# Weight pieces loaded over the place of their low halves, an attention head issued in pairs, late pieces spread out, and a branch moved ahead of the last stores

## The chip, the cores and the metric

One NeuronCore of a Trainium2 chip runs the whole program in one launch. The metric is the device time of one execution in microseconds (us), lower is better. The kernel before takes 930.59 us, the median of three runs (928.19 to 931.43).

## The reference

```python
# q, k, v, f_logit: [4 batches, 8 heads, 768 steps, 48]
f = 1.0 / (1.0 + np.exp(-f_logit))
for t in range(S):                       # gated linear attention
    state = f[:, :, t, :, None] * state + np.einsum('bhd,bhe->bhde', k[:, :, t], v[:, :, t])
    y[:, :, t] = np.einsum('bhd,bhde->bhe', q[:, :, t], state)
# x = y as 3072 tokens x 384
h = x @ w_in                             # first MLP, 384 -> 2048 -> 384
g = np.where(h >= 1, h, np.where(h <= -1, 0.0, (h + 1) ** 2 / 4.0))
x = g @ w_out
h = x @ w2_in                            # second MLP, same sizes
g = (a[0] + a[1]*h + a[2]*h**2 + a[3]*h**3) / (1.0 + abs(b[0])*abs(h) + abs(b[1])*h**2 + 1e-06)
out = g @ w2_out
```

## The kernel before, in words

All data are float32. A large product is made of three rounded ones: each operand is split into a high half (`_hi`, a rounding copy made by ScalarE, ACT) and a low half (`_lo`, the difference, made by VectorE, DVE, or GpSimd, POOL), and TensorE (PE) multiplies high by high, high by low and low by high. Nine matmuls of 128x512 make one tile of a hidden layer from the 384 inputs, and nine add one hidden tile to the three output sums.

**Attention** is cut in 24 items (6 chunks of 128 steps by 4 groups of head pairs). For item i: ACT makes the gate (`gate_steps`), DVE a running product (`scan`), ACT its logarithm and exponential as a first inverse (`invert`), DVE refines it (`newton`) and scales the queries (`scale_queries`), POOL scales the keys (`scale_keys`), PE makes the scores, DVE masks them (`mask`), PE makes the outputs, transposes the keys and makes the change of state (`scores`, `outputs`, `transposes`, `deltas`), ACT and DVE split the result into `x_hi` and `x_lo` (`round_y`, `rest_y`), and DVE adds to the state (`states`). Items 0 to 3, which complete the inputs of the first 512 tokens, run in a head that is written out by hand.

**The first MLP** follows in 96 steps n (6 blocks of 512 tokens by 16 hidden tiles). Step n issues `spline_first(n)` (nine matmuls into one of two banks), ACT's relu and square (`spline_in`), DVE's join (`spline_join`), ACT's high half (`spline_hi`), DVE's low half (`spline_lo`), and two steps later `spline_second(n)` (nine matmuls). Item 4 + n//4 of attention is spread over four steps (a window): `transposes(i)` and `scores(i)` stand behind `spline_first` of the first step, `outputs(i)` and `deltas(i)` behind that of the third. `transposes(i)` waits until DVE has added the state change of item i-1.

**Weights.** Each MLP's weights are 16 pieces of 384 KB. They stay in `w_hi` and `w_lo` for all blocks. A raw piece is loaded by a DMA that SyncE (SP) issues into one of two buffers `w_raw`, ACT rounds it into `w_hi` (`split_w1`, `split_w2`), and POOL subtracts into `w_lo` in three parts. A load waits until POOL has finished with its buffer. The second MLP's pieces go to the same `w_hi` and `w_lo`, each as soon as the first MLP has read the old piece for the last time, in its last block (n from LAST_BLOCK = 80): ten at the steps in `STEPS2`, and six late ones at the steps 0 to 5 of the second MLP.

**The second MLP** has 48 units (6 blocks by 8), each of two hidden tiles: unit n's step issues `rational_first(n)` (18 matmuls) and `rational_second(n-4)` (18); ACT, DVE and POOL work between them. At the steps 4, 5 and 6 of a block POOL also makes one third of the next block's `x_lo` (`split_x2`), and `rational_first` of the next block waits for all three.

Each engine runs its own program in order, and semaphores tie them together, so the order in which the code is written decides what stands behind a wait. At the end a flag tells whether the fast path was valid. PE, DVE, ACT and SP read it (`value_load`), and each jumps over a long general program (`general`) that does not run here.

Of the kernel before, what the change touches and what calls it, by code (L numbers as in the profile page):

```python
# [58 lines left out]
ORDER1 = [m + UNITS * out for m in range(UNITS) for out in range(2)]  # L59
# [9 lines left out]
X2_STEPS = [3, 4, 6]  # L69

# [37 lines left out]
def build(nc, qT, kT, fT, vT, fC, kC, qC, vC, w1, w2, a, b, outT):  # L108
# [3 lines left out]
    with ctx:  # L112
# [9 lines left out]
        w_lo = lay.tile("w_lo", PIECES * WPC, F32R)  # L122
        x_hi = lay.tile("x_hi", [P, KT, 2 * NB], F32R)
# [3 lines left out]
        w_raw = [lay.tile(f"w_raw{u}", WPC) for u in range(2)]  # L127
# [105 lines left out]
        w1_loaded = [sem(f"w1_loaded{r}") for r in range(2)]  # L233
        w1_hi_done = sem("w1_hi_done")
        w1_lo_done = sem("w1_lo_done")
        w2_loaded = [sem(f"w2_loaded{r}") for r in range(2)]
# [94 lines left out]
        def _(sp):  # L331
# [32 lines left out]
            def load_w1(k):  # L364
                if k >= 2:
                    sp.wait_ge(w1_lo_done, SPLITS * (k - 1))
                at = ORDER1[k] * WPC
                sp.dma_start(w_raw[k % 2][:, :], w1[:, at:at + WPC]).then_inc(w1_loaded[k % 2], 16)

            def load_w2(k):  # L370
                if k >= 2:
                    sp.wait_ge(w2_lo_done, SPLITS * (k - 1))
                else:
                    sp.wait_ge(w1_lo_done, SPLITS * PIECES)
                at = ORDER2[k] * WPC
                sp.dma_start(w_raw[k % 2][:, :], w2[:, at:at + WPC]).then_inc(w2_loaded[k % 2], 16)
# [54 lines left out]
            load_f(5)  # L431
            move_fourth(0)
# [4 lines left out]
            load_w1(2)  # L437
            load_q(5)
            load_w1(3)
            load_v(5)  # L440
            load_w1(4)
            sp.dma_start(a_bc[:, :], a.rearrange("(o a) -> o a", o=1).to_broadcast([P, 4])).then_inc(coef_loaded, 16)
            sp.dma_start(b_bc[:, :], b.rearrange("(o a) -> o a", o=1).to_broadcast([P, 2])).then_inc(coef_loaded, 16)
            for n in range(N1):
# [10 lines left out]
                if n + HEAD_PIECES + 2 < PIECES:  # L455
                    load_w1(n + HEAD_PIECES + 2)
                if n % TILES == LAG1 + 1 and n >= TILES:
                    store1(n // TILES - 1)
                t = n - (N1 - TILES)
# [7 lines left out]
            for k in range(len(STEPS2) + 2, PIECES):  # L467
                load_w2(k)
# [5 lines left out]
            store2(BLOCKS - 1)  # L474
            sp.wait_ge(flag_set, 1)
            flag = sp.value_load(okflag[0:1, 0:1], min_val=0, max_val=P)
            sp.wait_ge(stored2, 16 * KT * BLOCKS)
            with sp.If(flag < P):
                general.sync_program(sp, qT, kT, fT, vT, xT, x1T, w1, w2, outT)

        @block.gpsimd
        def _(pool):
# [26 lines left out]
            def split_w1(k):  # L509
                pool.wait_ge(w1_hi_done, k + 1)  # L510
                for part in range(SPLITS):
                    own = slice(part * WPC // SPLITS, (part + 1) * WPC // SPLITS)
                    at = slice(ORDER1[k] * WPC + own.start, ORDER1[k] * WPC + own.stop)
                    nc.gpsimd.tensor_tensor(w_lo[:, at], w_raw[k % 2][:, own], w_hi[:, at].bitcast(F32),
                                            ALU.subtract).then_inc(w1_lo_done, 1)

            def split_w2(k):
                m = ORDER2[k]
                pool.wait_ge(w2_hi_done, k + 1)
                if m < UNITS:  # L520
                    pool.wait_ge(h1_ready, N1 - TILES + UW * (m + 1))
                else:
                    pool.wait_ge(multiplied1, N1 - TILES + UW * (m - UNITS + 1))
                for part in range(SPLITS):
                    own = slice(part * WPC // SPLITS, (part + 1) * WPC // SPLITS)
                    at = slice(m * WPC + own.start, m * WPC + own.stop)
                    nc.gpsimd.tensor_tensor(w_lo[:, at], w_raw[k % 2][:, own], w_hi[:, at].bitcast(F32),  # L527
# [37 lines left out]
            split_w1(1)  # L565
            scale_keys(4)
            split_w1(2)
# [449 lines left out]
        def _(pe):  # L1017
# [179 lines left out]
            for n in range(N1):  # L1197
                i, stage = window_of(n)
                spline_first(n)
                if n == 0:  # L1200
                    deltas(3)
# [298 lines left out]
```

## Time and profile before

| | us |
|---|---|
| median of 3 runs | 930.59 |
| the profiled execution, its whole time | 931.32 |
| its span in the profile | 929.6 |
| PE busy | 894.3 (96%) |
| DVE busy | 666.1 (72%) |
| ACT busy | 632.3 (68%) |
| POOL busy | 277.8 (30%) |
| ACT's last operation begins | 922.78 |

The span is the time from the first instruction to the last in one profiled execution, and 1.7 us lie around it. A busy PE is not PE at its peak: matmuls overlap in the profile, so the distance from one start to the next says more than the busy time.

### The profile page before, as it was taken

The numbers are of one execution on the slowest core, as the hardware profiler recorded it, in microseconds if no ns is written. First come the engines' busy times: TensorE is split into PE (matmuls) and PEld (weight loads), VectorE is DVE, ScalarE is ACT, GpSimd is POOL, SyncE is SP. The second block draws the span as 40 slices with busy tenths as digits, with TensorE's granted clock in tenths as the row PEclk, the third lists the DMA queues.
The fourth block names the chain that finished last, engine by engine and source line by source line (L and its number), as shares of the span: only waits on it lengthen the run. The fifth ranks groups of instructions, "written<-read, shape, count | busy, mean of one in ns | idle before, by whom it ended". The sixth has DMA issues, their size and how long they took to land.

```text
span 929.6 us, 13243 instructions
## 1 busy us (share of the span) xinstructions
PE 894.3 (96%) x4786; PEld 737.5 (79%) x4786; DVE 666.1 (72%) x813; ACT 632.3 (68%) x821; POOL 277.8 (30%) x202
## 2 busy tenths in 40 slices
PE   4799999999999999999999998999999999999996
PEld 3577788888888888888888886888888888888884
DVE  7866656655655566565344799889899889889883
ACT  5566665556555655655577796888787888887881
POOL 3455500000010000000055487235344244353223
PEclk9699999999999999999999998999999999999999
DMA  6434313212211211110233221001001001000001
GB/s 190 117 96 133 103 35 97 58 35 62 59 35 36 85 55 49 58 37 1 69 102 88 83 68 35 1 35 34 0 34 34 23 11 34 34 0 0 34 0 38
DMA packets 27513, 48.72 MB, mean 52 GB/s; under 512 B 5312, under 2 KB 8384, under 8 KB 27456
## 3 DMA queue, kind: packets, MB, share of 16 engines
q1 hardware_dynamic: 27456, 48.00, 17.3%
q8 instruction: 31, 0.51, 0.2%
q14 instruction: 26, 0.21, 0.1%
HBM read 36.18 MB, written 9.44 MB: 49 GB/s over the span
## 4 chain that ended last, share of the span: by engine, by line
PE 79%; DVE 8%; ACT 5%; issue 4%; POOL 3%; POOLq 0%; DMA 0%; SPq 0%; DVEq 0%; ACTq 0%
PE acc L1121 18%; PE acc L1165 18%; PE h_pair L1104 17%; PE at_pair L1143 10%; PE h_pair L1143 10%; PE at_pair L1044 2%; DVE growth L838 2%; PE at_pair L1063 2%; PE at_pair L1058 2%; DVE g L909 1%; POOL g_lo L548 1%; POOL w_lo L527 1%; ACT t L656 1%; ACT t L653 1%; DVE guess L856 1%
## 5 line engine op out<-in xcount | busy, mean ns | idle before, releaser
L548 POOL TENSOR_TENSOR g_lo<-g,g_hi 128x1024 fp32r<-128x1024 f32 x48 | 116.7, 2432 | 222.9 <-DVE t L938 218.4
L909 DVE SCALAR_TENSOR_TENSOR g<-h_pair,t 128x512 f32<-128x512 f32 x96 | 66.4, 691 | 142.1 <-ACT t L656 141.9
L653 ACT ACTIVATE t<-h_pair,half 128x512 f32<-128x512 f32 x96 | 66.0, 688 | 101.1 <-PE h_pair L1104 99.9
L1104 PE MATMUL h_pair<-x_hi,w_hi 128*128 128x512 f32 x288 | 113.6, 394 | 2.8 <-DVE x_lo L902 2.5
L507 POOL TENSOR_TENSOR k_s<-k_in,growth 128x512 f32<-128x512 f32 x22 | 29.0, 1316 | 289.0 <-DVE growth L838 288.2
L1165 PE MATMUL acc<-g_hi,w_hi 128*128 128x512 f32 x288 | 112.5, 390 | 1.9 <-POOL g_lo L548 1.9
L1104 PE MATMUL h_pair<-x_hi,w_lo 128*128 128x512 f32 x288 | 112.9, 392 | 0.0
L1104 PE MATMUL h_pair<-x_lo,w_hi 128*128 128x512 f32 x288 | 112.8, 392 | 0.0
L1165 PE MATMUL acc<-g_lo,w_hi 128*128 128x512 f32 x288 | 112.1, 389 | 0.0
L1165 PE MATMUL acc<-g_hi,w_lo 128*128 128x512 f32 x288 | 112.1, 389 | 0.0
L1121 PE MATMUL acc<-g_hi,w_hi 128*128 128x512 f32 x264 | 107.5, 407 | 0.0
L663 ACT CAST g_hi<-g 128x512 fp32r<-128x512 f32 x88 | 54.6, 621 | 75.3 <-DVE g L909 75.2
L1121 PE MATMUL acc<-g_hi,w_lo 128*128 128x512 f32 x264 | 103.2, 391 | 0.0
L1121 PE MATMUL acc<-g_lo,w_hi 128*128 128x512 f32 x264 | 102.9, 390 | 0.0
L917 DVE TENSOR_TENSOR g_lo<-g,g_hi 128x512 fp32r<-128x512 f32 x88 | 63.0, 716 | 46.7 <-ACT g_hi L663 46.7
L929 DVE SCALAR_TENSOR_TENSOR s<-s,b_abs,g 128x1024 f32<-128x1024 f32 x48 | 66.6, 1388 | 37.8 <-ACT g L709 37.7
L527 POOL TENSOR_TENSOR w_lo<-w_raw,w_hi 128x256 fp32r<-128x256 f32 x48 | 48.1, 1030 | 69.9 <-ACT w_hi L647 66.3
L1104 PEld LDWEIGHTS h_pair<-x_hi,w_hi 128*128 128x128 f32 x288 | 54.5, 189 | 15.4 <-DVE x_lo L902 3.0
L953 DVE SCALAR_TENSOR_TENSOR g<-g,a_bc,t 128x1024 f32<-128x1024 f32 x48 | 65.5, 1364 | 0.0
L1165 PEld LDWEIGHTS acc<-g_hi,w_hi 128*128 128x128 f32 x288 | 54.1, 188 | 14.2 <-POOL g_lo L548 3.1
L1104 PEld LDWEIGHTS h_pair<-x_hi,w_lo 128*128 128x128 f32 x288 | 54.5, 189 | 11.5
L1104 PEld LDWEIGHTS h_pair<-x_lo,w_hi 128*128 128x128 f32 x288 | 54.5, 189 | 11.2
(142 smaller groups left out, 2053.9 us busy)
## 6 DMA issues: line engine op xcount, KB each, us to landing
w_raw<-w SPq DMA_DIRECT2D x32, 384.0 KB, 3.4
f_in<-fC SPq DMA_DIRECT2D x48, 96.0 KB, 2.9
k_in<-kC SPq DMA_DIRECT2D x48, 96.0 KB, 2.4
q_in<-qC SPq DMA_DIRECT2D x48, 96.0 KB, 2.3
mlp_out<-o_sb SPq DMA_DIRECT2D x18, 256.0 KB, 3.3
x_raw<-mlp_out SPq DMA_DIRECT2D x6, 768.0 KB, 4.4
outT<-o_sb SPq DMA_DIRECT2D x18, 256.0 KB, 2.0
v_in<-vC SPq DMA_DIRECT2D x22, 192.0 KB, 2.5
```

Source lines behind the costliest of these rows:

```text
L527: nc.gpsimd.tensor_tensor(w_lo[:, at], w_raw[k % 2][:, own], w_hi[:, at].bitcast(F32), ALU.subtract).then_inc(w2_lo_done, 1)
L548: nc.gpsimd.tensor_tensor(g2_lo[r][:, :, :], g2[r][:, :, :], g2_hi[r][:, :, :].bitcast(F32), ALU.subtract).then_inc(lo2_ready, 1)
L653: nc.scalar.activation(t1[n % 2][:, :], h1[n % 2], ACT.Relu, scale=0.5, bias=half[:, :]).then_inc(relu1_ready, 1)
L663: nc.scalar.copy(hi, g1[n % 2][:, :]).then_inc(hi1_ready, 1)
L909: nc.vector.scalar_tensor_tensor(out=g1[n % 2][:, :], in0=h1[n % 2], scalar=1.0, in1=t1[n % 2][:, :], op0=ALU.max, op1=ALU.min).then_inc(g ...
L917: nc.vector.tensor_tensor(lo, g1[n % 2][:, :], hi.bitcast(F32), ALU.subtract).then_inc(lo1_ready, 1)
L929: nc.vector.scalar_tensor_tensor(out=s, in0=s, scalar=b_abs[:, 1:2], in1=g, op0=ALU.mult, op1=ALU.add).then_inc(den_ready, 1)
L953: nc.vector.scalar_tensor_tensor(out=g_before, in0=g_before, scalar=a_bc[:, 0:1], in1=t_before, op0=ALU.add, op1=ALU.mult).then_inc(g2_rea ...
L1104: mm = nc.tensor.matmul(h1[n % 2], w[:, at:at + P], x[:, kt, cols], start=(kt == 0 and j == 0), stop=(kt == KT - 1 and j == 2))
L1121: mm = nc.tensor.matmul(acc[o][:, :], w[:, at:at + P], g, start=(t == 0 and j == 0), stop=(t == TILES - 1 and j == 2))
L1143: mm = nc.tensor.matmul(h2[m % 2][:, c * NB:(c + 1) * NB], w[:, at:at + P], x[:, kt, xcols], start=(k == 0), stop=(k == 3 * KT - 1))
L1165: mm = nc.tensor.matmul(acc[o][:, :], w[:, at:at + P], g[m % R2][:, c, :], start=(m == 0 and c == 0 and k == 0), stop=(last and c == UW - ...
```

## The change

It has four parts.

1. `w_raw` becomes one tensor at the same addresses as `w_lo`. Every piece has its own place and its own semaphore for the load. POOL subtracts in place. The first MLP's loads wait for nothing. A load of the second MLP's piece waits itself for the last reader of the old piece (`h1_ready` or `multiplied1`), where before ACT and POOL did that behind a load made earlier. `ORDER1` changes so that a piece of the first layer comes one place sooner in relation to its partner, and ACT's `split_w1` in the loop comes one step later.
2. The head is in pairs: items 2 and 3 go through scan, newton, mask, outputs and transposes side by side, and the first four steps n are written out by hand on ACT, DVE and PE, interleaved with items 4 and 5.
3. The six late pieces are split at the steps 0, 1, 2, 3, 7 and 8 of the second MLP (`LATE_PIECES`).
4. SP reads the flag ahead of the last block's stores and branches ahead of the wait for their landing; ACT reads the flag before the second MLP.

```diff
-ORDER1 = [m + UNITS * out for m in range(UNITS) for out in range(2)]
+ORDER1 = [0, 1, 8, 2, 9, 3, 10, 4, 11, 5, 12, 6, 13, 7, 14, 15]
+LATE_PIECES = {0: [10], 1: [11], 2: [12], 3: [13], 7: [14], 8: [15]}
...
         w_lo = lay.tile("w_lo", PIECES * WPC, F32R)
+        lay.at -= 4 * PIECES * WPC
+        w_raw = lay.tile("w_raw", PIECES * WPC)
...
-        w_raw = [lay.tile(f"w_raw{u}", WPC) for u in range(2)]
...
             def load_w1(k):
-                if k >= 2:
-                    sp.wait_ge(w1_lo_done, SPLITS * (k - 1))
...
             def load_w2(k):
-                if k >= 2:
-                    sp.wait_ge(w2_lo_done, SPLITS * (k - 1))
+                m = ORDER2[k]
+                if m < UNITS:
+                    sp.wait_ge(h1_ready, LAST_BLOCK + UW * (m + 1))
                 else:
-                    sp.wait_ge(w1_lo_done, SPLITS * PIECES)
...
+                    sp.wait_ge(multiplied1, LAST_BLOCK + UW * (m - UNITS + 1))
...
@@ sync
             load_f(5)
+            load_w1(2)
             move_fourth(0)
...
-                if t in (0, 1):
-                    load_w2(t)
-                if t in STEPS2:
-                    load_w2(STEPS2.index(t) + 2)
+                if t + 1 in STEPS2:
+                    load_w2(STEPS2.index(t + 1))
...
             store2(BLOCKS - 2)
-            store2(BLOCKS - 1)
             sp.wait_ge(flag_set, 1)
             flag = sp.value_load(okflag[0:1, 0:1], min_val=0, max_val=P)
+            store2(BLOCKS - 1)
+            with sp.If(flag < P):
+                sp.wait_ge(stored2, 16 * KT * BLOCKS)
+                general.sync_program(sp, qT, kT, fT, vT, xT, x1T, w1, w2, outT)
+
             sp.wait_ge(stored2, 16 * KT * BLOCKS)
-            with sp.If(flag < P):
-                general.sync_program(sp, qT, kT, fT, vT, xT, x1T, w1, w2, outT)
...
@@ gpsimd
-            late_pieces = range(len(STEPS2), PIECES)
-            for off, piece in enumerate(late_pieces):
-                rational_step(0, off, [piece])
-            run2(pool, rational_step, 1 + UNITS, UNITS + 2, done=len(late_pieces), peel=1)
+            for off in range(UNITS + 1):
+                rational_step(0, off, LATE_PIECES.get(off, ()))
+            run2(pool, rational_step, UNITS + 1, UNITS + 2, done=UNITS + 1, peel=1)
...
@@ scalar
-                if n + HEAD_PIECES < PIECES:
-                    split_w1(n + HEAD_PIECES)
+                if n <= PIECES - HEAD_PIECES:
+                    split_w1(n + HEAD_PIECES - 1)
...
+            act.wait_ge(flag_set, 1)
             flag = act.value_load(okflag[0:1, 0:1], min_val=0, max_val=P)
+            for off in range(UNITS + 1):
+                rational_step(0, off, LATE_PIECES.get(off, ()), ends_first=(off == LAG2 - 1))
+            run2(act, rational_step, UNITS + 1, UNITS + LAG2, done=UNITS + 1, peel=1)
...
@@ tensor
+            deltas(0)
             scores(2)
-            deltas(0)
+            scores(3)
             outputs(2)
+            outputs(3)
             transposes(2)
-            scores(3)
+            transposes(3)
             deltas(1)
-            outputs(3)
-            transposes(3)
             deltas(2)
-            due = 0
-            for n in range(N1):
+            spline_first(0)
+            deltas(3)
+            spline_first(1)
+            transposes(4)
+            spline_first(2)
+            spline_second(0)
+            scores(4)
+            spline_first(3)
+            second_half(4)
+            spline_second(1)
+            due = LAG1
+            for n in range(WINDOW, N1):
```

The order of ACT in the new head, from item 3 on, is invert(3), round_y(1), copy_keys(1), gate_steps(4), split_w1(0), split_w1(1), round_y(2), round_y(3), copy_keys(2), copy_keys(3), split_w1(2), gate_steps(5), spline_in(0), invert(4), spline_hi(0), spline_in(1), spline_hi(1), copy_keys(4), split_w1(3), spline_in(2), spline_hi(2), invert(5), split_w1(4), spline_in(3), spline_hi(3), round_y(4), gate_steps(6), split_w1(5).

What DVE does in the head, before, from the result of item 1 (`h_pair`) to that of item 3 (`at_bank`): `growth_86` is item 4's running product, L854 to L865 are item 3's queries.

```order
L902 TENSOR_TENSOR x_lo<-h_pair,x_hi 48x512 x2
L877 TENSOR_TENSOR probs_94<-acc,causal 128x512 x2
L854 TENSOR_TENSOR q_s_91<-growth_87,guess_89 128x512
L856 SCALAR_TENSOR_TENSOR guess_89<-q_s_91,guess_89 128x512
L865 SCALAR_TENSOR_TENSOR q_s_91<-guess_89,q_in_83 128x512
L902 TENSOR_TENSOR x_lo<-acc,x_hi 48x512 x2
L877 TENSOR_TENSOR probs_95<-at_bank,causal 128x512
L877 TENSOR_TENSOR probs_95<-acc,causal 128x512
L838 SCALAR_TENSOR_TENSOR growth_86<-growth_86,ends,zero 128x128 x4
L842 COPY ends<-growth_86 128x4
L902 TENSOR_TENSOR x_lo<-at_bank,x_hi 48x512 x2
```

And in the changed program, from item 3's queries on (each line number is 8 higher and each buffer number 1 lower):

```order
L862 TENSOR_TENSOR q_s_90<-growth_86,guess_88 128x512
L864 SCALAR_TENSOR_TENSOR guess_88<-q_s_90,guess_88 128x512
L873 SCALAR_TENSOR_TENSOR q_s_90<-guess_88,q_in_82 128x512
L885 TENSOR_TENSOR probs_93<-acc,causal 128x512 x2
L885 TENSOR_TENSOR probs_94<-at_bank,causal 128x512
L885 TENSOR_TENSOR probs_94<-acc,causal 128x512
L910 TENSOR_TENSOR x_lo<-h_pair,x_hi 48x512 x2
L910 TENSOR_TENSOR x_lo<-acc,x_hi 48x512 x2
L910 TENSOR_TENSOR x_lo<-at_bank,x_hi 48x512 x2
L899 TENSOR_TENSOR state_76<-state_76,at_pair 48x4x48 x2
L899 TENSOR_TENSOR state_73<-state_73,h_pair 48x4x48 x2
L846 SCALAR_TENSOR_TENSOR growth_85<-growth_85,ends,zero 128x128 x4
```

The three low halves of the inputs now stand together behind both masks, and item 4's running product stands behind them.

What POOL does in the steps 2 to 6 of the second MLP, before: `w_lo` is a weight piece, `x_lo` a third of the next block's inputs, `g_lo` a unit's low half.

```order
L548 TENSOR_TENSOR g_lo_119<-g_0_114,g_hi_118 128x1024
L527 TENSOR_TENSOR w_lo<-w_raw_56,w_hi 128x256 x3
L548 TENSOR_TENSOR g_lo_121<-g_1_115,g_hi_120 128x1024
L527 TENSOR_TENSOR w_lo<-w_raw_57,w_hi 128x256 x3
L548 TENSOR_TENSOR g_lo_123<-g_2_116,g_hi_122 128x1024
L527 TENSOR_TENSOR w_lo<-w_raw_56,w_hi 128x256 x3
L537 TENSOR_TENSOR x_lo<-x_raw,x_hi 128x512
L548 TENSOR_TENSOR g_lo_125<-g_3_117,g_hi_124 128x1024
L527 TENSOR_TENSOR w_lo<-w_raw_57,w_hi 128x256 x3
L537 TENSOR_TENSOR x_lo<-x_raw,x_hi 128x512
L548 TENSOR_TENSOR g_lo_119<-g_0_114,g_hi_118 128x1024
L537 TENSOR_TENSOR x_lo<-x_raw,x_hi 128x512
```

And in the changed program, from the third `g_lo` to step 8:

```order
L546 TENSOR_TENSOR g_lo_122<-g_2_115,g_hi_121 128x1024
L535 TENSOR_TENSOR x_lo<-x_raw,x_hi 128x512
L546 TENSOR_TENSOR g_lo_124<-g_3_116,g_hi_123 128x1024
L535 TENSOR_TENSOR x_lo<-x_raw,x_hi 128x512
L546 TENSOR_TENSOR g_lo_118<-g_0_113,g_hi_117 128x1024
L535 TENSOR_TENSOR x_lo<-x_raw,x_hi 128x512
L546 TENSOR_TENSOR g_lo_120<-g_1_114,g_hi_119 128x1024
L525 TENSOR_TENSOR w_lo<-w_raw,w_hi 128x256 x3
L546 TENSOR_TENSOR g_lo_122<-g_2_115,g_hi_121 128x1024
L525 TENSOR_TENSOR w_lo<-w_raw,w_hi 128x256 x3
```

The last two weight pieces have moved from the steps 4 and 5, where they stood ahead of the `x_lo` parts, to the steps 7 and 8, behind all of them.

## Rows read from the trace of the kernel before

**Rows 1.** The page: busy time by engine.

```profile
PE 894.3 (96%) x4786; PEld 737.5 (79%) x4786; DVE 666.1 (72%) x813; ACT 632.3 (68%) x821; POOL 277.8 (30%) x202
```

**Rows 2.** Windows: length, busy (count) of PE, PEld, DVE, ACT, POOL; granted clock, DMA.

```profile
18.95:38.40 19.45, 13.45 (x144) 10.51 (x144) 16.21 (x27) 11.66 (x20) 6.90 (x9) 0.71 0.39 106
560.00:580.00 20.00, 16.78 (x62) 13.33 (x61) 19.86 (x14) 12.15 (x12) 16.04 (x8) 0.84 0.13 39
```

**Rows 3.** Waits of PE: us in total, times, longest.

```profile
PE at_bank L1028 <- DVE state L891: 3.6, 3, 1.6
PE at_pair L1143 <- POOL x_lo L537: 3.2, 1, 3.2
PE h_pair L1104 <- DVE x_lo L902: 2.5, 2, 1.9
```

**Rows 4.** Chain that ended last, 18 to 43 us: start, us, what.

```profile
22.29 1.29 DVE growth L838 x4
...
33.94 2.59 DVE growth L838 x4
...
38.42 4.21 PE h_pair L1104 x9
```

**Rows 5.** The same chain, 44 to 62 us.

```profile
44.48 1.11 PE at_pair L1044 x16
...
47.91 2.46 DVE growth L838 x4
...
57.76 0.69 DVE q_s L854
...
60.66 0.68 DVE y_lo L898
```

**Rows 6.** The same chain in the second MLP, at 895 us.

```profile
895.50 4.09 PE h_pair L1143 x18
```

**Rows 7.** Timeline of SP and PE in the head.

```profile
24.86 3.76 SPq L387 DMA_DIRECT2D x_lo<-y_lo  x6
...
58.36 0.39 PE L1104 MATMUL h_pair<-x_hi,w_hi 128*128 128x512 f32 x1
...
62.12 0.63 PE L1028 MATMUL at_bank<-ident,k_s 128*128 128x128 f32 x4 [1.56 <-DVE state L891]
```

**Rows 8.** Timeline of POOL and PE, 541 to 575 us.

```profile
541.02 2.42 POOL L548 TENSOR_TENSOR g_lo<-g,g_hi 128x1024 fp32r<-128x1024 f32 x1 [2.52 <-DVE t L938]
...
549.74 2.41 POOL L548 TENSOR_TENSOR g_lo<-g,g_hi 128x1024 fp32r<-128x1024 f32 x1 [1.25 <-DVE t L938]
552.11 5.09 POOL L527 TENSOR_TENSOR w_lo<-w_raw,w_hi 128x256 fp32r<-128x256 f32 x3
...
559.40 2.41 POOL L548 TENSOR_TENSOR g_lo<-g,g_hi 128x1024 fp32r<-128x1024 f32 x1
...
571.41 2.24 POOL L537 TENSOR_TENSOR x_lo<-x_raw,x_hi 128x512 fp32r<-128x512 f32 x1
...
574.05 0.79 PE L1143 MATMUL at_pair<-x_hi,w_hi 128*128 x1 [3.22 <-POOL x_lo L537]
```

**Rows 9.** Lines 478, 112 and 406, instructions: ns min/median/max, first and last start.

```profile
L478 SPq COMPARE_BRANCH  x1: 50/50/50, 926.6 to 926.6; - x1
...
L112 ACTq DRAIN  x1: 80/80/80, 926.8 to 926.8; - x1
L112 SPq DRAIN  x1: 48/48/48, 929.3 to 929.3; - x1
...
L406 SPq DMA_DIRECT2D outT<-o_sb x18: 332/332/360, 609.8 to 923.4; - x18
```

**Rows 10.** Landing of line 376's loads, and timeline of PE and ACT.

```profile
DMA to landing us min/median/max: 2.9/3.3/5.4
...
474.05 0.39 PE L1104 MATMUL h_pair<-x_hi,w_hi 128*128 128x512 f32 x1
...
480.77 0.83 ACT L647 CAST w_hi<-w_raw 128x768 fp32r<-128x768 f32 x1
```

More of the change, by code:

```diff
@@ L232, in build @@
         coef_loaded = sem("coef_loaded")
[L233 removed]
+        w1_loaded = [sem(f"w1_loaded{k}") for k in range(PIECES)]
         w1_hi_done = sem("w1_hi_done")
         w1_lo_done = sem("w1_lo_done")
[L236 removed]
+        w2_loaded = [sem(f"w2_loaded{k}") for k in range(PIECES)]
         w2_hi_done = sem("w2_hi_done")
@@ L511, in split_w1 @@
                 for part in range(SPLITS):
-                    own = slice(part * WPC // SPLITS, (part + 1) * WPC // SPLITS)
-                    at = slice(ORDER1[k] * WPC + own.start, ORDER1[k] * WPC + own.stop)
-                    nc.gpsimd.tensor_tensor(w_lo[:, at], w_raw[k % 2][:, own], w_hi[:, at].bitcast(F32),
+                    at = slice(ORDER1[k] * WPC + part * WPC // SPLITS, ORDER1[k] * WPC + (part + 1) * WPC // SPLITS)
+                    nc.gpsimd.tensor_tensor(w_lo[:, at], w_raw[:, at], w_hi[:, at].bitcast(F32),
                                             ALU.subtract).then_inc(w1_lo_done, 1)
@@ L779, in _ @@
             gate_steps(5)
-            for n in range(N1 + LAG1):
+            spline_in(0)
+            invert(4)
+            spline_hi(0)
+            spline_in(1)
+            spline_hi(1)
+            copy_keys(4)
+            split_w1(3)
+            spline_in(2)
+            spline_hi(2)
+            invert(5)
+            split_w1(4)
+            spline_in(3)
+            spline_hi(3)
+            round_y(4)
+            gate_steps(6)
+            split_w1(5)
+            for n in range(WINDOW, N1 + LAG1):
                 i, stage = window_of(n) if n < N1 else (None, None)
@@ L964, in _ @@
             mask(1)
+            scan(3)
             rest_y(0)
@@ L967, in _ @@
             scale_queries(2)
-            scan(3)
-            rest_y(1)
-            mask(2)
             newton(3)
             scale_queries(3)
+            mask(2)
+            mask(3)
+            rest_y(1)
             rest_y(2)
-            mask(3)
-            scan(4)
             rest_y(3)
             states(0)
-            newton(4)
-            scale_queries(4)
             states(1)
+            scan(4)
             states(2)
             states(3)
-            for n in range(N1):
+            spline_join(0)
+            newton(4)
+            spline_lo(0)
+            scale_queries(4)
+            spline_join(1)
+            mask(4)
+            spline_lo(1)
+            scan(5)
+            spline_join(2)
+            spline_lo(2)
+            newton(5)
+            scale_queries(5)
+            spline_join(3)
+            rest_y(4)
+            states(4)
+            spline_lo(3)
+            for n in range(WINDOW, N1):
                 i, stage = window_of(n)
@@ L1205, in _ @@
                     second_half(i)
-                if n >= LAG1 and n not in HOLD:
+                if n not in HOLD:
                     spline_second(due)
```

68 lines of the change are left out of this document (26 added, 42 removed).

## The prediction

> **What bounds the kernel now.** I first read the page. PE is busy 894.3 of 929.6 us [rows 1], so nearly the whole time is its matmuls, and at most some 35 us can be won from its gaps, plus what it loses at its lower clock. Then the windows, to see where it isn't full: from 18.95 to 38.40 us PE is busy 13.45 of 19.45 at a mean granted clock of 0.71, and from 560 to 580 it is busy 16.78 of 20 at 0.84 [rows 2]. Its waits give names to these places [rows 3]: a last low half of the inputs in the head (2.5, DVE), three waits for a state (3.6, DVE), one for a third of `x_lo` before block 1 of the second MLP (3.2, POOL). Between 130 and 550 us, and from 580 us to the last units, PE has no wait over 0.4 us. So only three places count: the head up to some 125 us, the change of block at 571 us, and the end. Elsewhere other engines have time to spare.
>
> **Price of the lower clock.** Nine matmuls of 512 columns take 4.21 us at 38.42 [rows 4], while eighteen take 4.09 at 895 us [rows 6]: 0.43 to 0.47 against 0.227 us each, the levels of 1.2 and 2.4 GHz. At the change of block PE stood still for 3.2 us and came back at the lower level [rows 2, 8]. I read 14 slow matmuls there in the trace, 0.2 us too long each: 2.8 us. So a gap of over 3 us costs itself and 2.8 more. Gaps of up to 1.6 us between 60 and 125 us [rows 3, 7] did not lower the clock.
>
> **The head, up to the first spline matmul (before at 38.42).** In the 19.45 us from the end of item 1's mask at 18.95 DVE is busy 16.21 [rows 2]. The new order takes item 4's running product out of this stretch, 2.59 us [rows 4] and 0.5 for the copy behind it, and nothing of POOL's weight subtraction meets item 3's query operation, which took 0.6 longer than the same one of item 2. That leaves 12.5 us, and since both scans and queries now stand ahead of the masks, DVE hardly waits: 18.95 + 12.5 + 0.7 for handoffs is 32.2. Two other things come due near it. The 12 small transfers of `move_fourth` end their issue at 28.6 [rows 7]; one microsecond later because of y's later low half, and 2 us to land, is 31.7. And PE must make `deltas(1)`, wait for ACT's copy of item 2's keys (0.6) and make `deltas(2)` before the spline, which ends at 32.5 if its clock is full and at 34.6 if it is not. I take 32.7, 5.7 us sooner. PE's own work from 20 to 33 us is now closer together (the gap of 2.4 us before item 2's outputs goes), so I take it that the full clock holds. From the first spline step to the fifth (58.36, [rows 7]) are 19.94 us, 2.8 of them due to the lower clock. At full clock the fifth would begin at 32.7 + 17.1 = 49.8: 8.6 us sooner.
>
> **The head, item 5.** Then `transposes(5)` waits for the state of item 4. Before, that was ready 16.5 us after item 4's scores ended at 45.6 (1.56 us late) [rows 5, 7]. The new chain is item 4's mask, the low half of step 1, item 5's scan, step 2's join, item 5's inverse on ACT, a weight piece, step 3 on ACT and DVE, y's halves and the state. Against before, item 5's queries (57.76 to 60.66, 2.9 us [rows 5]) are off it, and the scan is not met by a weight subtraction: 1.29 instead of 2.46 [rows 4, 5]. That is 16.5 - 2.9 - 1.1 = 12.5. But PE now has only two spline steps, one second step and item 4's outputs behind these scores, 3 x 2.04 + 2.45 = 8.6 us. So it waits 3.9, 2.3 more than before. By what happened at 571 us such a gap lowers the clock: 2.8 more. Later waits for states and for block 1's inputs (0.8, 1.2 and 0.6) should go, since ACT and DVE are 5 us or more ahead: 2.6 back. Sum of the head: 8.6 - 2.3 - 2.8 + 2.6 = 6.1. My chain has more handoffs than I counted, so I take 5.5. Bounds: 1.4 if the clock is lost early as well (2.8 and the 1.9 of the later start), 8.9 if it is never lost.
>
> **Loads without a ring.** The first MLP's pieces now come early. SP's waits for POOL go, and one wait of ACT of 1.2 us at 80 us; both lie beside full PE, so nothing. In the last block a load starts only when the old piece's reader is done. The tightest: `spline_first(85)` has issued when 86 begins at 474.05, and ACT rounds the piece at 480.77: 6.7 us of cover, less 0.2, against 2.9 to 5.4 to land [rows 10]. The other nine have as much or more by the same reckoning, the late ones over 8 us. Cost 0, hidden by three spline steps; with the cover gone ACT stands, and PE follows after two more steps (4 us). The POOL operation in place isn't in the trace: between nothing and, at worst, a little longer; POOL is busy only 30% of the span [rows 1], so 0. ACT's early read of the flag (some 1 us) lies in front of unit 0, while PE has held second steps to do: 0.
>
> **The change of block.** PE has used up its work at 574.05 - 3.22 = 570.8 and waits for the third `x_lo` part, ready at 573.65 [rows 8]. In the steps 4 and 5 POOL has 2.4 + 5.1 + 2.3 = 9.8 us to do and starts its `g_lo` every 9.66, while PE's step is 36 matmuls, 8.17 us [rows 6, 8]. The two weight pieces (5.09 each) leave these steps. Then the first part starts at 552.2, and two steps later, at PE's pace, the third: 552.2 + 16.3 + 2.3 = 570.8, just in time. DVE alone would be faster (its six operations of a unit, 1.2 to 1.3 each, make 7.5), which gives 569.5. At the pace that a step with a piece had earlier, 8.72 (541.02 to 549.74 [rows 8]), it would be 571.9 and PE would wait 1.1, too short for the clock. So of 3.4 + 2.8 = 6.2 us between 5.1 and 6.2 come back; I take 6.0. Pieces 14 and 15 then fall in the steps 7 and 8, needed by PE at 10 and 11. They stretch DVE's step to 8.7 at most, 0.5 over PE's, twice, and PE runs a unit ahead: 0.
> The Trainium skill (SBUF — State Buffer, Who interferes with whom) says that a DVE operation with two SBUF inputs and a POOL operation that reads SBUF exclude each other. By that rule moving a piece moves the loss with it; whether that shows on PE is the rival below.
>
> **The end.** SP's compare and branch is at 926.6, after the wait for the last landing, and its next instruction at 929.3 [rows 9]: the jump over the general program takes 2.7 us that nothing hides. Now the branch follows the last store's issue (923.4 + 0.4 [rows 9]) and the landing at 926.6 covers it. ACT's jump, begun at 923.8 beside the same stores, ended at 926.8 [rows 9], so SP may be ready then too; the program then ends 2.4 earlier, 2.7 at best, 2.0 with PE's 3.6.
> The Trainium skill (Advanced Engine Details and Errata, Control Flow Timing) puts a compare-and-branch at about 108 ns; by it this part would give 0.1. Its page Runtime: NRT & Kernel Launch (Instruction fetch mechanics) says that a taken branch to a far target must fetch it first; by this rule, the trace agrees.
>
> **Sum.** 5.5 + 6.0 + 2.4 = 13.9. The profiled execution took 931.32 in all, 0.7 over the median of the runs; off the median it gives 916.7, off its own 917.4. I say 917.0. Under 0.3% (2.8 us) a measurement here can't tell from no change.
>
> **Rivals.**
> - The head gives little: the clock falls near 27 us as before and again at item 5. Speaking for it are the gaps that stay before item 2's scores. Head 1.4, sum 9.8: 921. Chance 0.18.
> - The clock is kept in the head altogether, because the wait before item 5 is nearer 2 than 4 us. Head 8.9, sum 17.3: 913.5. Chance 0.12.
> - Contention moves but stays: DVE, 19.86 of 20 us busy at 560 to 580 [rows 2], is the true pace there and not POOL, and the third part is late by 3 us as before. Then the change of block gives 0: 922.8. Against it is that DVE's operations are stretched only while POOL works. Chance 0.1.
> - The end gives nothing since another engine's closing instruction also stands at 929: 919.3. ACT's was at 926.8, which speaks against it. Chance 0.07.
> - Slower: the loads of the last block come too late. SP issues in order, so one load held up holds all behind. It decides when a load takes over 6.5 + 4 us from its reader's end; each such stall over 3 us costs PE about 6 with the clock, and from three of them the gains are gone: 935 with four. Chance 0.04.
> - Head and change of block both disappoint, and only the end stays: 928, about no change. Chance 0.05.
> The forecast has 0.44.
>
> **Numbers.** From 912.5, under the good clock, to 924, over the contention rival, is 0.85 or so of this. Faster by over 0.3%: 0.91; within: 0.05; slower: 0.04.
>
> **What would show it.** First spline matmul near 33 us and the clock at 1.0 there; `transposes(5)` waiting some 4 us at about 54 to 58; the first matmul of block 1 of the second MLP without a wait over 1.1 us, at full clock; SP's branch near 924 and its DRAIN under 927.5; no wait of ACT on `w_raw` from 460 us on. The prediction is wrong if PE's order in the head makes it wait for ACT's key copies beyond 36 us, if a new wait of over 2 us shows in the last block, or if the third `x_lo` part still ends last.

## The result, and the profile after

The changed kernel takes 920.28 us (median of 4 runs, 918.66 to 921.05), the kernel before in the same session 930.88 (928.19 to 931.43): ratio 0.989, 95% interval 0.9865 to 0.9914. That is 10.6 us less, where 13.9 were forecast; 917.0 was the forecast time, and the range of 912.5 to 924 holds the result. The profiled executions are 11.7 us apart (span 929.6 and 917.9).

The page of the changed kernel, engine by engine, answers to [rows 1]: PE has 6 us less to do (it spends less time at its low clock), and 29.5 us of gaps in place of 35.3.

```profile
PE 888.4 (97%) x4786; PEld 733.2 (80%) x4786; DVE 663.6 (72%) x813; ACT 632.2 (69%) x821; POOL 276.8 (30%) x202
```

Its waits of PE answer to [rows 3] (us in total, times, longest). The wait for the third `x_lo` part at the change of block has fallen from 3.2 to 0.5. The three waits for a state are now almost one, of 3.5, and the longest wait for a low half of the inputs has a new place, block 1.

```profile
PE at_bank L1050 <- DVE state L899: 3.7, 2, 3.5
PE h_pair L1126 <- DVE x_lo L910: 2.3, 2, 2.0
...
PE at_pair L1165 <- POOL x_lo L535: 0.5, 1, 0.5
```

The timeline of PE shows where in the head these stand: the first spline matmul, the fifth spline step, the transposes of items 5, 6 and 7, and block 1's first matmul.

```profile
32.56 0.50 PE L1126 MATMUL h_pair<-x_hi,w_hi 128*128 128x512 f32 x1 [0.35 <-DVE x_lo L910]
...
50.79 0.39 PE L1126 MATMUL h_pair<-x_hi,w_hi 128*128 128x512 f32 x1
...
56.51 1.09 PE L1050 MATMUL at_bank<-ident,k_s 128*128 128x128 f32 x4 [3.52 <-DVE state L899]
...
79.63 0.60 PE L1050 MATMUL at_bank<-ident,k_s 128*128 128x128 f32 x4
...
100.54 0.63 PE L1050 MATMUL at_bank<-ident,k_s 128*128 128x128 f32 x4 [0.17 <-DVE state L899]
...
121.25 0.50 PE L1126 MATMUL h_pair<-x_hi,w_hi 128*128 128x512 f32 x1 [2.00 <-DVE x_lo L910]
```

The same four matmuls `x4` take 0.63 us at 100.54 and 1.09 at 56.51: the clock fell during the gap ahead of them. The windows say the same (columns as in [rows 2]): the window from 20 to 40 us is at full clock, and the two after it are not.

```profile
20.00:40.00 20.00, 16.12 (x184) 12.62 (x182) 19.07 (x36) 15.14 (x26) 9.03 (x11) 1.00 0.56 155
40.00:60.00 20.00, 16.48 (x118) 13.42 (x117) 12.93 (x23) 13.18 (x22) 8.57 (x10) 0.88 0.51 143
60.00:80.00 20.00, 20.00 (x116) 16.62 (x115) 12.92 (x21) 10.08 (x17) 9.17 (x10) 0.95 0.65 189
...
560.00:580.00 20.00, 19.46 (x86) 15.80 (x85) 19.83 (x16) 18.13 (x18) 12.47 (x7) 1.00 0.12 39
```

At the change of block, the timeline of POOL and PE answers to [rows 8]: POOL now waits for DVE ahead of each `g_lo`, and makes the third `x_lo` part 0.54 us (with the handoff) after PE's work ran out.

```profile
562.63 2.41 POOL L546 TENSOR_TENSOR g_lo<-g,g_hi 128x1024 fp32r<-128x1024 f32 x1 [3.65 <-DVE t L946]
565.00 2.27 POOL L535 TENSOR_TENSOR x_lo<-x_raw,x_hi 128x512 fp32r<-128x512 f32 x1
...
567.67 0.49 PE L1165 MATMUL at_pair<-x_hi,w_hi 128*128 x1 [0.54 <-POOL x_lo L535]
```

At the end, lines 479, 115 and 409 answer to [rows 9] (ns min/median/max, first and last start). SP branches at 914.5, right behind the issue of the last store. When the landing comes, only a short branch and its DRAIN are left: SP's next instruction begins 0.65 us behind the landing, at 917.47, where it was 2.78 before. From the last store to the end of the span it takes 3.8 us, where it took 6.2. Not all of these 2.4 us belong to the branch: the last store landed 2.68 us after its issue began, where the one before took 3.14.

```profile
L479 SPq COMPARE_BRANCH  x1: 50/50/50, 914.5 to 914.5; - x1
...
L115 ACTq DRAIN  x1: 80/80/80, 916.4 to 916.4; - x1
L115 SPq COMPARE_BRANCH  x1: 43/43/43, 917.5 to 917.5; - x1
L115 SPq DRAIN  x1: 13/13/13, 917.6 to 917.6; - x1
...
L409 SPq DMA_DIRECT2D outT<-o_sb x18: 332/332/360, 601.1 to 914.1; - x18
```

The loads of the second MLP's weights land in 3.0 to 4.0 us, and no line of ACT's rounding shows a wait for one:

```profile
L640 ACT CAST w_hi<-w_raw x16: 826/832/852, 460.6 to 575.4; 128x768 fp32r<-128x768 f32 x16
```

### The profile page after: what moved, and what is told of

It is laid out like the page before. It is cut to its first block, busy times and chain, and to the rows that moved or that the text cites. A ratio compares the mean times of both kernels' runs of the same rounds, so it can differ in the third digit from the quotient of the medians.

```text
span 917.9 us, 13209 instructions
## 1 busy us (share of the span) xinstructions
PE 888.4 (97%) x4786; PEld 733.2 (80%) x4786; DVE 663.6 (72%) x813; ACT 632.2 (69%) x821; POOL 276.8 (30%) x202
## 4 chain that ended last, share of the span: by engine, by line
PE 82%; DVE 8%; ACT 4%; issue 4%; POOL 1%; POOLq 0%; DMA 0%; DVEq 0%; SPq 0%; ACTq 0%
PE acc L1143 19%; PE acc L1187 18%; PE h_pair L1126 18%; PE at_pair L1165 10%; PE h_pair L1165 10%; PE at_pair L1066 3%; PE at_pair L1085 2%; DVE growth L846 2%; PE at_pair L1080 2%; DVE g L917 1%; POOL g_lo L546 1%; PE at_bank L1050 1%; DVE probs L885 1%; ACT t L649 1%; ACT t L646 1%
## 5 line engine op out<-in xcount | busy, mean ns | idle before, releaser
L937 DVE SCALAR_TENSOR_TENSOR s<-s,b_abs,g 128x1024 f32<-128x1024 f32 x48 | 69.4, 1445 | 31.9 <-ACT g L702 31.8
L961 DVE SCALAR_TENSOR_TENSOR g<-g,a_bc,t 128x1024 f32<-128x1024 f32 x48 | 63.6, 1325 | 0.0
L1187 PEld LDWEIGHTS acc<-g_hi,w_lo 128*128 128x128 f32 x288 | 54.1, 188 | 11.4
```

The source lines that it names most:

```text
L937: nc.vector.scalar_tensor_tensor(out=s, in0=s, scalar=b_abs[:, 1:2], in1=g, op0=ALU.mult, op1=ALU.add).then_inc(den_ready, 1)
L961: nc.vector.scalar_tensor_tensor(out=g_before, in0=g_before, scalar=a_bc[:, 0:1], in1=t_before, op0=ALU.add, op1=ALU.mult).then_inc(g2_rea ...
L1187: mm = nc.tensor.matmul(acc[o][:, :], w[:, at:at + P], g[m % R2][:, c, :], start=(m == 0 and c == 0 and k == 0), stop=(last and c == UW - ...
```

## The experiments

Each was timed against the kernel before in the same session, in 4 to 12 runs; the ratio is to that. The kernel before had medians of 930.88, 929.12, 929.49 and 930.34 us in the four sessions (the changed kernel in the first; late_back, branch_back, piece15 and filler in the second; old_head, second_first, early_splits and sf_es in the third; the rest in the fourth), so I also cut every profiled execution at the same three instructions. *Head* ends with the first spline matmul of block 1; *middle* with the first `at_pair<-x_hi,w_hi` behind the change of block; *second MLP* with the start of the last 18 matmuls; *tail* is the rest of the span. Middle and second MLP agree to some hundredths of a microsecond wherever code and clock are the same (to 0.2 in the two kernels that have no wait ahead of block 1), so these two stretches price their parts well. The head does not: the changed kernel, branch_back and late_back have the same code there and end it at 121.25, 121.52 and 122.41. Nor do the ratios tell piece15, filler, second_first and early_splits (0.9886 to 0.9891) from the changed kernel (0.989). What is said of gains among these rests on one trace of each and on medians of different sessions.

| kernel | median us | ratio and interval | head | middle | second MLP | tail |
|---|---|---|---|---|---|---|
| before | 930.9 | | 124.98 | 449.07 | 344.32 | 11.2 |
| changed | 920.3 | 0.989 (0.9865 to 0.9914) | 121.25 | 446.42 | 341.44 | 8.8 |
| inplace_only | 929.5 | 1.0001 (0.9986 to 1.0017) | 124.96 | 449.04 | 343.00 | 10.8 |
| late_only | 925.6 | 0.9957 (0.9943 to 0.9972) | 124.94 | 446.38 | 341.40 | 10.9 |
| branch_only | 927.8 | 0.9988 (0.9974 to 1.0003) | 123.22 | 449.07 | 341.41 | 9.3 |
| branch_back | 921.7 | 0.9922 (0.9905 to 0.9938) | 121.52 | 446.35 | 341.42 | 10.7 |
| late_back | 925.0 | 0.9953 (0.9939 to 0.9968) | 122.41 | 449.09 | 343.02 | 8.7 |
| old_head | 923.5 | 0.9933 (0.9913 to 0.9952) | 125.53 | 446.35 | 341.44 | 8.8 |
| piece15 | 917.9 | 0.9891 (0.9873 to 0.9909) | 119.52 | 446.38 | 341.44 | 8.7 |
| filler | 918.7 | 0.9889 (0.987 to 0.9907) | 119.78 | 446.35 | 341.41 | 8.7 |
| second_first | 918.3 | 0.9886 (0.9861 to 0.991) | 118.57 | 446.36 | 341.43 | 8.6 |
| early_splits | 919.9 | 0.989 (0.9865 to 0.9914) | 122.12 | 446.20 | 341.63 | 8.7 |
| sf_es | 917.4 | 0.9875 (0.9848 to 0.9902) | 119.20 | 446.23 | 341.43 | 8.7 |
| sf_p15 | 916.1 | 0.9869 (0.9847 to 0.9891) | 117.72 | 446.42 | 341.41 | 8.8 |

### Late pieces: late_back, and late_only with inplace_only

late_back is the changed kernel with

```
-LATE_PIECES = {0: [10], 1: [11], 2: [12], 3: [13], 7: [14], 8: [15]}
+LATE_PIECES = {0: [10], 1: [11], 2: [12], 3: [13], 4: [14], 5: [15]}
```

> The changed kernel with the late pieces 14 and 15 back at the steps 4 and 5 of the second MLP, all else as changed. Theory of the third part of x_lo: POOL's two weight pieces stand ahead of the x_lo parts again, PE waits some 3.2 us for the third part near 570 us, comes back at the lower clock, and the time rises from 920.3 by 5.5 us to about 925.8. Rival (the loads without a ring made the change of block quicker, not the place of the two pieces): under 1.5 us more than 920.3, PE's wait under 1 us.

By the medians it took 4.7 us more than the changed kernel. In the traces 4.25 us belong to the change of block (2.67 in the middle, 1.58 in the second MLP). Its timeline of PE and a window (columns as in [rows 2]) show the old wait and a fall of the clock:

```profile
571.50 0.79 PE L1165 MATMUL at_pair<-x_hi,w_hi 128*128 x1 [3.20 <-POOL x_lo L535]
...
570.00:580.00 10.00, 8.50 (x30) 6.93 (x31) 8.52 (x7) 6.93 (x7) 3.50 (x2) 0.83 0.27 79
```

From the other side, inplace_only is the kernel before with nothing but the raw pieces in place, their loads doing the waiting. late_only adds the late pieces to it (and with them ACT's early read of the flag and SP's ahead of the last store, with the branch where it was). Of inplace_only's edit, one place of several:

```
...
-                nc.scalar.copy(w_hi[:, at], w_raw[k % 2][:, :]).then_inc(w2_hi_done, 1)
+                nc.scalar.copy(w_hi[:, at], w_raw[:, at]).then_inc(w2_hi_done, 1)
...
```

> The kernel before with the raw pieces in place and the loads doing the waiting, nothing else changed: the old head, the splits of pieces 14 and 15 at items 4 and 5 of the last block, the branch last. My prediction gave this part 0: 929 to 931 us, the same as the kernel before within 0.3%. Rival: the ring did cost something (a load that waited for its slot, or a slower subtraction in place), then 2 us or more off in either direction.

> The kernel before with the raw pieces in place and pieces 14 and 15 split at items 7 and 8 of the last block; head and branch as before. If the change of block is worth what late_back gave up (4.7 us) to the 5.5 us of the traces, this takes 924.0 to 925.2 us against 929.5 to 930.9 for the kernel before. By the prediction's 6.0: 923.5 to 925. If late pieces are worth less without the new head: above 926.

In place alone is worth nothing, to within 1.6 us. The late pieces then give 4.0 (929.5 to 925.6), and 4.26 in middle and second MLP of the traces, with the old head as well as with the new. The contention rival, by which the third part stays late, falls: with the pieces at steps 7 and 8 DVE is still 19.83 of 20 us busy between 560 and 580, but PE waits 0.5 instead of 3.2. On DVE the loss did move: in the changed kernel three of its operations beside the piece at step 7 (574.34 to 579.4) take 1.65 to 1.76 us where they take 1.21 to 1.29 without POOL. PE has no wait behind that.

### The end: branch_back and branch_only

branch_back is the changed kernel with the wait for the stores ahead of the branch again; branch_only is the kernel before with this wait behind it, its flag still read after the last store. The edit of branch_back:

```
+            sp.wait_ge(stored2, 16 * KT * BLOCKS)
             with sp.If(flag < P):
-                sp.wait_ge(stored2, 16 * KT * BLOCKS)
                 general.sync_program(sp, qT, kT, fT, vT, xT, x1T, w1, w2, outT)
-            sp.wait_ge(stored2, 16 * KT * BLOCKS)
```

> The changed kernel with SP's branch back behind the wait for the last landing, all else as changed (ACT reads its flag early as changed). Theory of the jump: SP's next instruction comes 2.7 us after the branch and nothing hides it; time up by 2.4 us to 922.7, and the branch at the landing, the closing DRAIN 2.7 later. Rival (another engine's closing instruction sets the end): up by under 0.5 us.

> The kernel before with the wait for the last stores behind SyncE's branch, nothing else changed. The chain at the end gives 2.4 us: 927.1 to 928.5. branch_back gave up only 1.4 of them (921.69 against 920.28); if that is the true worth, 928.1 to 929.5. In the trace the last store is to end 3.7 us before the span's end instead of 6.2. Rival: nothing, 929.5 to 930.9.

The medians say 1.4 (branch_back) and 2.6 us (branch_only); the ratio of branch_only says 1.1, with an interval from a gain of 2.4 to a loss of 0.3. The traces are sharper: the tail is 10.7 to 11.2 us in the four kernels with the late branch and 8.6 to 9.3 in the ten with the early one. The changed kernel against branch_back (8.75 and 10.74) and branch_only against the kernel before (9.27 and 11.22) both give 2.0. So the branch is worth some 2 us. In branch_only the last store's line reads:

```profile
L406 SPq DMA_DIRECT2D outT<-o_sb x18: 332/332/362, 605.1 to 918.7; - x18
```

From there to its end at 923.0 are 4.3 us, 1.9 less than before. It branches at 920.02, 0.9 us after the store's issue and later than the changed kernel does, and its next instruction comes at 922.57: 2.55 us after the branch and 0.88 after the landing, so here a part of the jump still shows.

### The head as a whole: old_head

The changed kernel with the old order of the first items on all engines, the old `ORDER1` and the old places of the splits in the loop. The first lines of its edit:

```
-ORDER1 = [0, 1, 8, 2, 9, 3, 10, 4, 11, 5, 12, 6, 13, 7, 14, 15]
+ORDER1 = [m + UNITS * out for m in range(UNITS) for out in range(2)]
...
```

> The changed kernel with the head of the kernel before: the old order of the first eight scans and of the first window, all else as changed (raw pieces in place, late pieces, early branch, new change of block). If the head is worth what the two traces show at block 1's first matmul (124.98 before, 121.25 changed), this takes 3.7 us more than the changed kernel: about 924.0 us; block 1's first matmul again near 125.0 and the wait ahead of it 0.56 instead of 2.00. If the head's worth is the 5.5 us of the prediction: 925.8. If the head was worth nothing and the gain lies elsewhere: 920.3.

The new head is worth 3.3 us by medians and 3.7 to 4.3 by the traces of before, old_head and the changed kernel. Over all executions it is about 3: the five with the old order end the head at 124.7 in the mean (123.22 to 125.53), the three with the changed kernel's head at 121.7 (121.25 to 122.41). It is not 5.5. Block 1's first matmul has its short wait again:

```profile
125.53 0.50 PE L1093 MATMUL h_pair<-x_hi,w_hi 128*128 128x512 f32 x1 [0.56 <-DVE x_lo L891]
```

### Why the head gives less: filler, piece15, early_splits, second_first

First, is it the clock lost at `transposes(5)`? filler puts 14 matmuls whose result nobody reads into the gap ahead of them.

```
+                if n == WINDOW:
+                    for _ in range(14):
+                        nc.tensor.matmul(at_pair[:, NB:2 * NB], w_hi[:, 0:P], x_hi[:, 0, 0:NB], start=True, stop=True)
```

> The changed kernel with 14 matmuls of 512 columns more, whose result nobody reads, behind spline_first(4), in the 3.5 us in which PE waits for the state of item 4; they only keep PE busy. Theory of the clock: the fall of the granted clock near 55 us goes, PE does transposes(5), scores(5) and the second step behind them 2.8 us sooner. Theory of the chain: ACT and DVE set the start of block 1, so the wait there grows from 2.0 to about 3.5 us and only 0.5 to 1.5 us of the 2.8 are left: 919.3. Rival (PE alone sets the pace, all 2.8 come back): 917.5. If the gap does not cause the fall, the clock falls all the same.

```profile
57.56 0.63 PE L1050 MATMUL at_bank<-ident,k_s 128*128 128x128 f32 x4 [0.30 <-DVE state L899]
...
119.78 0.50 PE L1126 MATMUL h_pair<-x_hi,w_hi 128*128 128x512 f32 x1 [2.00 <-DVE x_lo L910]
```

The clock is kept there. From `transposes(5)` to block 1 it takes 62.2 us, 2.5 less than the changed kernel's 64.7, though item 5 came a microsecond later. (0.7 of this microsecond is older than the filler: its first spline matmul stands at 33.24, at a lower clock ahead of it.) So most of a lost clock reaches block 1; that ACT and DVE swallow it, which I had held possible, is not so. The size of the loss varies: over the same stretch late_back takes 63.8 and branch_back 64.9 us, behind the same gap of 3.5. That is 1.5 to 2.7 us. The 2.00 us wait before block 1 is the same to the hundredth in four executions that reach it between 119.78 and 122.41. So it is made within the last window, and what PE gains or loses earlier does not change it. The changed kernel's chain there:

```profile
112.99 0.82 ACT w_hi L634
113.81 0.59 ACT t L646
...
116.50 1.24 issue
117.74 0.69 DVE q_s L862
...
119.79 0.68 DVE x_lo L910
```

A rounding of a weight piece stands in it: the changed loops split piece 15 at n = 13, one step later than before. It costs 0.82 us on ACT. It costs 0.66 more on DVE: POOL scales item 8's keys only behind its subtraction of this piece, at 115.98 to 117.27, and beside that DVE's low half of a step takes 1.35 us. Before, POOL was idle then and the same operation took 0.69. These 1.48 us are what the wait has grown by (1.44). The low half before and in the changed kernel:

```profile
120.86 0.69 DVE L917 TENSOR_TENSOR g_lo<-g,g_hi 128x512 fp32r<-128x512 f32 x1 [0.69 <-ACT g_hi L663]
```

```profile
116.47 1.35 DVE L925 TENSOR_TENSOR g_lo<-g,g_hi 128x512 fp32r<-128x512 f32 x1 [0.69 <-ACT g_hi L656]
```

piece15 splits piece 15 at n = 14 instead of 13; early_splits spreads the pieces so that none is split from n = 12 on.

```
+SPLITS1 = {1: [3], 2: [4], 3: [5], 4: [6], 5: [7, 8], 6: [9, 10], 7: [11], 8: [12], 9: [13], 10: [14], 11: [15]}
```

> The changed kernel with the last piece of the first MLP (piece 15) split one step later, at n = 14 behind round_y(7) on ACT and on POOL, instead of n = 13. Theory of the chain of ACT and DVE: in the window before block 1 the change has put one more piece (0.82 us on ACT, and a DVE low half stretched by 0.66 us) on the chain that ends in x_lo for block 1, where PE now waits 2.0 us; with the piece behind it the wait falls to about 0.5 us and the time to 918.8. Rival (the wait is for the transfers of move_fourth or for PE's own results): wait stays near 2.0, time 920.3.

> The extra raw pieces are split on items 5, 6 and so on up to 15 with two on items 5 and 6, so that none is split in the last window (items 12 to 15). One theory: the split of piece 13 to 15 beside the last scans makes the 2.00 us wait before block 1; then that wait falls to 0.2 to 0.5 us and the time to about 918.5 us. Rival: the pieces move the load from one window to another and a new wait stands before transposes(6) or (7), with 920.3 or more. With the extra piece moved alone the wait was 1.14, so under 1.14 is wanted here.

The same instruction in piece15, then `transposes(6)` and `transposes(7)` in early_splits:

```profile
119.52 0.50 PE L1130 MATMUL h_pair<-x_hi,w_hi 128*128 128x512 f32 x1 [1.14 <-DVE x_lo L914]
```

```profile
81.57 0.63 PE L1053 MATMUL at_bank<-ident,k_s 128*128 128x128 f32 x4 [0.38 <-DVE state L902]
...
103.56 0.63 PE L1053 MATMUL at_bank<-ident,k_s 128*128 128x128 f32 x4 [1.24 <-DVE state L902]
```

piece15 takes 0.86 of the 2.00 us away. The rest of the growth is the same piece in its new place: POOL's subtraction, now at 116.85, meets DVE's last operation on the queries, which takes 1.23 us where it took 0.69 before.

```profile
122.91 0.69 DVE L865 SCALAR_TENSOR_TENSOR q_s<-guess,q_in 128x512 f32<-128x512 f32 x1
```

```profile
116.92 1.23 DVE L877 SCALAR_TENSOR_TENSOR q_s<-guess,q_in 128x512 f32<-128x512 f32 x1
```

These 0.54 us and the old wait of 0.56 make 1.10 of the 1.14. (piece15's head ends 1.73 us sooner than the changed kernel's; the other 0.9 us are its clock behind `transposes(5)`, which fell for a shorter time.) early_splits takes the whole wait before block 1 away, and 1.45 us more than in the changed kernel stand in front of the two transposes: the wait follows the pieces from window to window. Its time is that of the changed kernel.

second_first fills the gap ahead of `transposes(5)` with work that is due anyway.

```
+                if n == WINDOW:
+                    spline_second(due)
+                    due += 1
...
-                if n not in HOLD:
+                if n not in HOLD and n != WINDOW:
```

> At scan 4 TensorE does the second spline product of item 2 ahead of the transposes and scores of item 5, so that 2.04 us of useful work lie in the 3.5 us gap ahead of transposes(5). My theory: the gap shrinks to about 1.5 us, the clock does not fall at 55, and 2.0 + 2.0 to 2.8 us come forward, less what the wait before block 1 grows by; about 916.3 us, wait before block 1 2.0 or more. Rival: the last window's chain on ScalarE and VectorE, not TensorE, sets block 1's start; then the wait before block 1 grows by the whole 4 us and the time is 920.3.

```profile
54.78 0.47 PE L1143 MATMUL acc<-g_hi,w_hi 128*128 128x512 f32 x1 [1.68 <-POOL w_lo L517]
...
97.86 0.63 PE L1050 MATMUL at_bank<-ident,k_s 128*128 128x128 f32 x4 [1.24 <-DVE state L899]
...
118.57 0.50 PE L1126 MATMUL h_pair<-x_hi,w_hi 128*128 128x512 f32 x1 [1.96 <-DVE x_lo L910]
```

The gap shrinks from 3.52 to 1.68 us and the clock stays full. What is left of it stands ahead of the moved product, which waits for the low half of a weight piece; `transposes(5)` follows without a wait. The head ends 2.7 us sooner, at 118.57; 2.0 us come back by the median, half of what I expected, and 1.07 of the rest stands at 97.86, where the wait for a state grew from 0.17 to 1.24.

### Together: sf_es and sf_p15

> Both edits, the second spline product of item 2 ahead of transposes(5) and no split in the last window. If the two gains are independent, 2.0 to 4.0 us from the filled gap and 1.5 to 1.8 from the wait before block 1: about 915.0 us (914.5 to 916.8), wait before block 1 under 1 us. If both buy the same slack on the last window's chain, it equals the better one alone, about 916.5 to 918.

> The changed kernel with the second spline product of item 2 ahead of transposes(5), and with piece 15 split one item later than piece 14's successor stood (at n = 14 instead of 13). Alone the first gave 918.3, the second 917.9, against 920.3. If their gains add: 915.9 us, the wait before block 1 1.1 us, no fall of the clock near 55. If both use the same slack: 917.9 to 918.3.

sf_es waits 1.93 ahead of `transposes(6)` and loses the clock behind that. sf_p15 is the better one: 916.07 (916.00 to 917.92), by medians 4.2 us under the changed kernel and 14 under the one before. All its four runs lie under all four of the changed kernel (918.66 and more), though in another session; the ratios, 0.9869 and 0.989, put only 2.0 us between them, and their intervals overlap. Its granted clock in the head, and its two late waits:

```profile
20.00:40.00 20.00, 16.18 (x183) 12.71 (x184) 19.07 (x36) 15.15 (x25) 9.03 (x11) 1.00 0.56 158
40.00:60.00 20.00, 18.32 (x132) 14.80 (x132) 13.76 (x25) 13.19 (x22) 8.59 (x10) 1.00 0.46 137
```

Against the changed kernel its head ends 3.5 us sooner, the sum of second_first's 2.7 and the 0.86 of wait that piece15 saves: these two gains add. Three of its four runs lie within 0.1 us of each other.

## Why the prediction was right, and where it was off

- **The sign and the three places** were right. The cuts add up: head 3.73, middle 2.65, second MLP 2.88, tail 2.47, in all 11.7, which is the difference of the profiled executions.
- **First spline matmul:** 32.56 against 32.7, at clock 1.00. The step of DVE, the transfers and PE's deltas was right in its sum. That the full clock holds there was partly luck. Nine executions have this code up to that matmul: in five it begins between 32.56 and 32.70, in the others at 33.24, 33.66, 33.81 and 34.56. The last is late_back, at a mean clock of 0.83 from 20 to 40 us, and is the 34.6 that the prediction named for a clock that is not full:

```profile
34.56 0.50 PE L1126 MATMUL h_pair<-x_hi,w_hi 128*128 128x512 f32 x1
...
20.00:40.00 20.00, 15.91 (x168) 12.91 (x165) 17.55 (x32) 13.56 (x22) 9.32 (x11) 0.83 0.56 160
```

- **Fifth step:** 50.79 against 49.8, 1 us too hopeful: I took 17.1 us for the stretch by PE's old work at full clock, and it took 18.2.
- **`transposes(5)`:** a wait of 3.52 against 3.9, and the clock fell, as argued from the gap at 571 us. By the filler it cost 2.5, against 2.8; in late_back it cost 1.5.
- **The step that failed** is "Later waits for states and for block 1's inputs (0.8, 1.2 and 0.6) should go, since ACT and DVE are 5 us or more ahead: 2.6 back". The 0.79 before item 6 went, the 1.24 before item 7 fell to 0.17, and the 0.56 before block 1 grew to 2.00: 0.4 back instead of 2.6. I looked at ACT and DVE at the start of the windows and not at what the new order of splits puts into the last one. Piece 15 at n = 13 is the cause of the 1.44: 0.82 on ACT and 0.66 in a DVE operation that POOL stretches. piece15 brings back 0.86 and leaves 0.54 in another stretched operation. The old 0.56 goes only where no piece at all is split in the last window (early_splits), and then a wait of the same size turns up in earlier windows: no placement tried is free.
- **Loads without a ring (the two `w_raw` buffers in turn): 0.** inplace_only gives 1.0001 for the whole part. No wait of ACT on a load shows in the last block. The slower rival falls.
- **The change of block:** 6.0 forecast; 5.5 between the two profiled executions (2.65 of wait and 2.88 of clock), 4.7 and 4.0 by the medians. The wait was right: the third part comes 0.54 late where I had it just in time, and pieces 14 and 15 at steps 7 and 8 cost nothing. The clock's term was mis-sized: 2.8 is what one execution lost, and the next section shows that it is 0, 1.6 or 2.9.
- **The end:** 2.4 forecast, 2.4 between the profiled executions, about 2 over all of them. That the first two agree is luck: some 2.0 are the jump that the landing now covers, the rest is a landing that took 2.68 us instead of 3.14. The Trainium skill (Advanced Engine Details and Errata, Control Flow Timing) gives some 108 ns for a compare-and-branch; the rows have 50 ns for the branch itself and then 2.5 to 2.8 us until SP's next instruction when it jumps over the long program (before 2.77, inplace_only 2.66, branch_back 2.49). Its page Runtime: NRT & Kernel Launch (Instruction fetch mechanics), which has a far target fetched first, agrees with them; no row shows the fetch itself.
- **Of the rivals,** "the head gives little" (921) is nearest in time but not in mechanism: in the profiled execution the clock did hold to 55 us. In late_back it fell early as well, as this rival has it. The result lies between it and the forecast, 3.3 us over the latter: 1.8 of the head by the two profiled executions, some 1.3 to 2 of the clock at the change of block by the medians.

## What to carry to other kernels

A gap on the bounding engine that also costs the clock is worth filling with a step that is due anyway. Work of no use kept the clock here too, but its gain of 1.5 us in the trace is within what runs of one kernel differ by. When a step is moved out of one window, list what every helper engine then does in the window that ends last; a saving forecast from "they are ahead by now" is a guess until that is done. Where medians scatter by more than the effect, cut the traces at the same instructions: stretches with the same code and clock agree to hundredths and price each part by itself. Where the clock differs, one trace is one draw.

## What the runs showed of the hardware

**The same gap doesn't always cost the clock.** PE's wait at the change of block is 3.20 to 3.22 us in four kernels. What followed differed. The windows and PE's rows behind the wait in the kernel before, in inplace_only and in branch_only, whose code there is alike:

```profile
570.00:580.00 10.00, 6.78 (x18) 5.07 (x17) 9.93 (x8) 4.91 (x5) 6.04 (x3) 0.67 0.27 79
```

```profile
574.00 0.49 PE L1131 MATMUL at_pair<-x_hi,w_hi 128*128 x1 [3.21 <-POOL x_lo L529]
...
570.00:580.00 10.00, 6.79 (x23) 5.18 (x22) 9.93 (x8) 4.88 (x6) 6.00 (x3) 0.83 0.26 79
```

```profile
572.29 0.49 PE L1145 MATMUL at_pair<-x_hi,w_hi 128*128 x1 [3.21 <-POOL x_lo L539]
...
570.00:580.00 10.00, 7.71 (x34) 6.40 (x35) 9.93 (x8) 7.42 (x7) 4.31 (x2) 1.00 0.25 79
```

In the kernel before the second MLP took 344.32 us, in inplace_only and late_back 343.00 and 343.02, in branch_only 341.41, as in all kernels without the wait. So one and the same gap costs 2.9, 1.6 or nothing besides itself.

**The head varies in the same way.** Two kernels with the old order of the head spent the stretch from 20 to 40 us at 0.63 (inplace_only) and 0.88 (branch_only), and branch_only's head ended 1.7 us sooner for it:

```profile
20.00:40.00 20.00, 13.64 (x134) 10.75 (x131) 17.15 (x31) 12.02 (x20) 7.47 (x9) 0.63 0.51 143
```

```profile
20.00:40.00 20.00, 13.65 (x149) 10.71 (x149) 18.45 (x32) 13.00 (x21) 8.77 (x10) 0.88 0.44 123
```

The new head varies too, as late_back's first spline matmul shows. The 26 runs of the kernel before in one session reach from 926.24 us at a mean clock of 0.993 to 932.21 at 0.983. The mean clock accounts for most of their scatter (the squared correlation with the time is 0.78), and a price read from one execution's slow matmuls is one draw from it.
